# Attention steps merged into units of a head pair and half the queries, in a kernel that hides attention beside an MLP

## The chip, the core and the metric

One core of one Trainium2 chip runs the kernel. The metric is device time in microseconds (us). TensorE (PE) multiplies, ScalarE (ACT), VectorE (DVE) and GpSimd (POOL) do the elementwise work, SyncE (SP) issues all DMAs. All data are float32; the MLPs run as float32r products of high and low parts.

## The reference

Attention in two forms on q, k, v of shape (4 batches, 8 heads, 576 positions, 64), then two MLPs on 2304 x 512:

```python
q_d, k_d, v_d = (t.reshape(B, H, 144, 4, D).mean(axis=3) for t in (q, k, v))
out_d = softmax(q_d @ k_d.T / 8) @ v_d              # pooled, repeated 4 times along the positions
mask = abs(pos[:, None] - pos[None, :]) < 4
out_local = softmax(where(mask, q @ k.T / 8, -1e9)) @ v
x = (repeat(out_d, 4) + out_local) -> (2304, 512)
h = x @ w_in;  x2 = (max(h, 0) + alpha * min(h, 0)) @ w_leaky    # 512 -> 2048 -> 512
xn = x2 / rms(x2) * rms_g
y = (silu(xn @ w_gate) * (xn @ w_val)) @ w_out                   # 512 -> 1536 -> 512
```

## The kernel before

Four engines run hand-written queues that meet through semaphores. The program has these stages:

1. The first stage: attention of batch 0 by `first_order` (L1036), while SP loads w_in and w_leaky and ACT, POOL and DVE split them into a high and a low part (`piece_hi`, `piece_lo`).
2. `first_mlp` for batches 0 to 2, in a loop of three rounds (L1047). A round has 2 halves of 16 chunks. A chunk is `up` (12 matmuls, L993) and `down` (12 matmuls, L1007, two chunks behind). So a round has 64 slots, each with 12 MLP matmuls; an even slot has `up`, an odd one `down`. Ahead of a slot's MLP matmuls stand the attention steps of the next batch that `steps[s]` gives it. ACT and DVE walk the same slots: at an even slot the attention steps, then `chunk_relu` or `chunk_leaky`; at an odd one the attention steps, then `chunk_hi` or `chunk_lo`.
3. `first_mlp` for batch 3 without attention, with the weights of the second MLP coming in.
4. `second_mlp` (L1072, L1087), six blocks.

Attention has lettered steps. A (per head pair, 4 parts): transposes of q and k, copied to `qkT` by ACT (L565); DVE pools them into `qkd` (L742). B (per head, 2 parts): scores of 5 windows of 120 queries x 128 keys (L952) and of the pooled form (L955); DVE adds the mask and takes maxima (L750 to L765). P and E: exponentials on ACT (L571, L579). F: division by the sums on DVE (L770 to L777). C (per head, 2 parts): transposes of the probabilities (L961, L965), copied to `pT` and `pdT` by ACT (L586 to L591). D (per head, 2 parts): products with v (L975, L980), scaled by ACT (L597) and added into `xpair` by DVE (L789). B has 64-row operands, rows 0 to 63 for an even head and 64 to 127 for an odd one; D has 64-column results, and again a half of the partitions for each head.

Beside the MLP only PSUM banks 6 and 7 are free for attention. `in_banks` deals them out in turn, and a step that fills a bank waits until the step that filled it before has been drained (`drained`). In the first stage eight banks are dealt. The steps that fill banks (64 in a batch) are spread over slots 8 to 62 in the order of `STEPS`:

```python
        for step in order:
            steps[SLOT0 + n * (SLOT1 - SLOT0) // (len(bank_of) - 1)].append(step)
            n += 1 if USES[step[0]] and n < len(bank_of) - 1 else 0
```

Of the kernel before, what the change touches and what calls it, by code (L numbers as in the profile page):

```python
# [5 lines left out]
def attention_into_two_mlps_kernel(nc: bass.Bass, q, k, v, w_in, w_leaky, alpha, w_gate, w_val, w_out, rms_g, out):  # L6
# [23 lines left out]
    NW = 5  # L30
    QW = 120
    KSTART = [(S - P) // (NW - 1) * i for i in range(NW)]
    QSTART = [0] + [s + 4 for s in KSTART[1:-1]] + [S - QW]
    QFIRST = [0] + [KSTART[i] + QW for i in range(NW - 1)]
    QOWN = [b - a for a, b in zip(QFIRST, QFIRST[1:] + [S])]
    SPLIT = 3
    NSPLIT = sum(QOWN[:SPLIT])
    SDH = SD // 2
    PR = S // 6
# [26 lines left out]
    SPLIT_X_AFTER = ("C", 7, 1)  # L66
# [21 lines left out]
    with ctx:  # L88
# [16 lines left out]
        mask = sb("mask", [QW, NW, P], f32, part1)  # L105
# [3 lines left out]
        vwin = sb("vwin", [P, 2, NW, 2, D], f32, part1)  # L109
        v4 = sb("v4", [SDH, 4, FACTOR, D], f32, part1)  # L110
        vd = sb("vd", [SDH, 2, 4, D], f32, part1)
        sm = sb("sm", [QW, 2, NW, P], f32, part1)
        pd = sb("pd", [SDH, 2, 2, SD], f32, part1)
        pT = sb("pT", [P, NW * QW], f32, part1)
        pdT = sb("pdT", [SDH, 2, SD], f32, part1)
        negmax = sb("negmax", [QW, 4, NW], f32, part1)
        negmaxd = sb("negmaxd", [SDH, 4, 4], f32, part1)
        sums = sb("sums", [QW, 4, NW + 2], f32, part1)
        rsum = sb("rsum", [QW, NW + 2], f32, part1)
        od = sb("od", [P, SD], f32, part1)  # L120
# [5 lines left out]
        sm_first = sb("sm_first", [QW, 2, NW, P], f32, part0)  # L126
        pd_first = sb("pd_first", [SDH, 2, 2, SD], f32, part0)
        pT_first = sb("pT_first", [P, NW * QW], f32, part0)
        pdT_first = sb("pdT_first", [SDH, 2, SD], f32, part0)
# [30 lines left out]
        banks = [ctx.enter_context(nc.psum_tensor(f"bank{i}", [P, 512], f32)) for i in range(8)]  # L160
# [9 lines left out]
        s_consts = sem("s_consts")  # L170
        s_chain = sem("s_chain")
# [10 lines left out]
        s_drained = {kind: sem(f"s_drained_{kind}") for kind in "ACD"}  # L182
        s_drained_b = [sem(f"s_drained_B{j}") for j in range(2)]
        s_qkT = sem("s_qkT")
        s_qkd = sem("s_qkd")
        s_masked = sem("s_masked")
# [3 lines left out]
        s_exp = sem("s_exp")  # L190
        s_guard = sem("s_guard")
# [60 lines left out]
        USES = {"A": 4, "B": 2, "C": 2, "D": 2, "P": 0, "E": 0, "F": 0}  # L252
# [4 lines left out]
        def in_banks(order, ring):  # L257

            fills = [step for step in order if USES[step[0]]]
            return {step: (ring[n % len(ring)], fills[n - len(ring)] if n >= len(ring) else None)  # L260
                    for n, step in enumerate(fills)}
# [6 lines left out]
        for step in first_order:  # L268
            if step[0] == "F" or step[::2] == ("B", 1):
                PIECES_AFTER[step] = (n, n + 1)  # L270
                n += 2
# [6 lines left out]
        def bank(b, kind, i, j):  # L278
            return banks[(first_bank_of if isinstance(b, int) and b == 0 else bank_of)[kind, i, j][0]]


# [9 lines left out]
        def probs_of(b, i):  # L291

            buf = (i - H + 2) % depth(b, "sm")
            return (sm[:, buf], pd[:, buf], buf) if buf < 2 else (sm_first[:, buf - 2], pd_first[:, buf - 2], buf)
# [9 lines left out]
        def probsT_of(b, i):  # L304

            return ((pT, pdT), (pT_first, pdT_first))[(H - 1 - i) % depth(b, "pT")]
# [6 lines left out]
        def filled(eng, b, kind, i, j):  # L313

            eng.wait_ge(s_filled[kind], USES[kind] * ((PAIRS if kind == "A" else H) * b + i) + j + 1)

        def drained(eng, b, kind, i, j):

            if kind == "B":
                eng.wait_ge(s_drained_b[j], H * b + i + 1)  # L320
            else:
                eng.wait_ge(s_drained[kind], USES[kind] * ((PAIRS if kind == "A" else H) * b + i) + j + 1)

# [10 lines left out]
        def _(sp):  # L334
# [17 lines left out]
            def load_qk(b, p, t):  # L352

                n0, pair = H * b + 2 * p, PAIRS * b + p
                later(sp, s_filled["A"], 4 * pair - 2 + 2 * t)
                for e in range(2):
                    sp.dma_start(qk_tok[:, t, :, e, :], (qf, kf)[t][bass.ds(n0 + e, 1), :, :]
                                 .rearrange("n (p r) d -> p (n r) d", r=6)).then_inc(s_qk_in[t], 16)

            def load_v(b, p):  # L360
# [7 lines left out]
                later(sp, s_filled["D"], 4 * pair - 4)  # L368
                for i in range(NW):
                    sp.dma_start(vwin[:, p % 2, i, :, :],  # L370
                                 vf[bass.ds(n0, 2), KSTART[i]:KSTART[i] + P, :].rearrange("n p d -> p n d")
                                 ).then_inc(s_v_in[p % 2], 16)

            def store_pair(b, p):
                drained(sp, b, "D", 2 * p + 1, 1)
                sp.dma_start(x_dram[bass.ds(b * DM + p * P, P), :], xpair_of(b, p)[:, :]).then_inc(s_x_out, 16)
# [17 lines left out]
            def load_block2(i):  # L394
                if isinstance(i, int) and i == 0:
                    sp.wait_ge(s_x2_out, 16 * -(-TB2 // TB1) + BEGUN)
                    drained(sp, B - 1, "D", H - 1, 1)
# [12 lines left out]
            def after_step(b, kind, i, j, more=True):  # L410
# [3 lines left out]
                if (kind, i % 2, j) == ("D", 1, 1):  # L414
# [62 lines left out]
        def _(pool):  # L477
# [6 lines left out]
            pool.memset(sums[:, :], 1.0).then_inc(s_consts, 1)  # L484
# [4 lines left out]
            for i in range(NW):  # L489
                off = QSTART[i] - KSTART[i]  # L490
                pool.affine_select(out=mask[:, i, :], in_=mask[:, i, :], compare_op=ALU.is_gt, fill=NEG,
                                   base=FACTOR + off, pattern=[[-1, P]], channel_multiplier=1
                                   ).then_inc(s_chain, 1)
            for i in range(NW):
                off = QSTART[i] - KSTART[i]
                pool.wait_ge(s_chain, 3 + i)
                pool.affine_select(out=mask[:, i, :], in_=mask[:, i, :], compare_op=ALU.is_gt, fill=NEG,
                                   base=FACTOR - off, pattern=[[1, P]], channel_multiplier=-1
# [13 lines left out]
            def v_sums(b, p):  # L512
                pair = PAIRS * b + p
                pool.wait_ge(s_v4_in, 32 * (pair + 1) if isinstance(pair, int) else 32 * pair + 32)
                later(pool, s_filled["D"], 4 * pair - 4)
# [9 lines left out]
            for kind, i, j in first_order:  # L525
# [3 lines left out]
                if (kind, i % 2, j) == ("D", 1, 1) and i // 2 + 2 < PAIRS:  # L529
# [9 lines left out]
        def _(act):  # L539
# [5 lines left out]
            def piece_hi(n):  # L545
                wait_piece(act, n)
                i = n if n < Q1 else n - Q1
                if n >= Q1:
                    if i < Q1:
                        act.wait_ge((s_h, s_g_used)[i % 2], C1 * (NB1 - 1) + i // 2 + 1 + BEGUN)  # L550
                    elif i == Q1:
                        drained(act, B - 1, "D", H - 1, 1)
                act.activation(wpiece(i, 0), ring_slot(n)[1], ACT.Copy).then_inc(s_whi, 1)

            def attention(b, kind, i, j):
                n = H * b + i
                qkT, qkd = qk_of(b, i if kind == "A" else i // 2)
                sm, pd, buf = probs_of(b, i)
                pT, pdT = probsT_of(b, i)
                if kind == "A":  # L560

                    later(act, s_filled["B"], 4 * (PAIRS * b + i + 1 - depth(b, "qkT")))
                    filled(act, b, kind, i, j)
                    t, r0 = j // 2, 3 * (j % 2)
                    act.activation(qkT[:, t, :].rearrange("p (a r) -> p r a", r=6)[:, r0:r0 + 3, :],  # L565
                                   bank(b, kind, i, j)[:, 0:3 * PR].rearrange("p (r a) -> p r a", r=3),
                                   ACT.Copy, scale=SCALE if t == 0 else 1.0).then_inc(s_drained["A"], 1)
                if kind == "P":
                    act.wait_ge(s_dmax, n + 1)
                    for c in range(2):  # L570
                        last = act.activation(pd[:, c, :],  # L571
                                              bank(b, "B", i, 1)[0:SDH, P + SD * c:P + SD * (c + 1)],
                                              ACT.Exp, bias=negmaxd[:, buf, 2 + c:3 + c], scale=1.0 / FACTOR ** 2,
                                              accum_out=sums[0:SDH, buf, NW + c:NW + c + 1])
                    last.then_inc(s_drained_b[1], 1)
                if kind == "E":
                    act.wait_ge(s_max, n + 1)
                    for w in range(NW):
                        last = act.activation(sm[:, w, :], sm[:, w, :], ACT.Exp,  # L579
                                              bias=negmax[:, buf, w:w + 1], accum_out=sums[:, buf, w:w + 1])  # L580
                    last.then_inc(s_exp, 1)
                if kind == "C" and j == 0:

                    later(act, s_filled["D"], 2 * (n + 1 - depth(b, "pT")))
                    filled(act, b, kind, i, j)
                    act.activation(pT[:, 0:4 * QW], bank(b, kind, i, j)[:, 0:4 * QW], ACT.Copy  # L586
                                   ).then_inc(s_drained["C"], 1)
                if kind == "C" and j == 1:
                    filled(act, b, kind, i, j)
                    act.activation(pT[:, 4 * QW:5 * QW], bank(b, kind, i, j)[:, 0:QW], ACT.Copy)  # L590
                    act.activation(pdT[:, :, :], bank(b, kind, i, j)[0:SDH, QW:QW + 2 * SD], ACT.Copy  # L591
                                   ).then_inc(s_drained["C"], 1)
                if kind == "D" and j == 0:
                    e = i % 2
                    later(act, s_drained["D"], 2 * n - 2)
                    filled(act, b, kind, i, j)
                    act.activation(od[D * e:D * e + D, :], bank(b, kind, i, j)[D * e:D * e + D, NSPLIT:NSPLIT + SD],  # L597
                                   ACT.Copy, scale=1.0 / FACTOR).then_inc(s_od, 1)

            def split_x(b, half, tiles=range(KT)):  # L600
                blk = 2 * b + half
                for t in tiles:
# [4 lines left out]
                    if half == 0 and t >= KT - depth(b, "xpair"):  # L607
                        drained(act, b, "D", 2 * t + 1, 0)
# [119 lines left out]
        def _(dve):  # L728
# [6 lines left out]
            def attention(b, kind, i, j):  # L735
                n = H * b + i
# [394 lines left out]
```

## Time and profile before

| | |
|---|---|
| median of 3 runs | 1099.6 us (1097.94 to 1099.8) |
| span of the profiled execution | 1098.4 us |
| first stage | to about 81 us |
| three rounds with attention | 81.1 to 232.6, 233.1 to 382.9, 384.7 to 532.9 us |
| the MLP alone, then the second MLP | from 532.9 us |
| PE busy | 1067.3 us, 97% |
| DVE, ACT, POOL busy | 493.8, 471.9, 100.5 us |

The profiled execution lies 1.2 us below the median. PE is the bound wherever it is busy all the time; the table's ends of the rounds are read from the chain of work.

### The profile page before, as it was taken

Reading aid. Unit: us, or ns where it says so; the run is one execution under the profiler, and the core shown is the slowest. Engines: PE = TensorE matmul, PEld = TensorE weight load, DVE = VectorE, ACT = ScalarE, POOL = GpSimd, SP = SyncE. Lnnn points to the kernel's source line nnn. Section 1 sums busy time; section 2 is a strip of 40 time slices with the busy share of each in tenths; the row PEclk is TensorE's granted clock in tenths of the full one; section 3 lists DMA queues with packets and bytes.
Section 4 is the critical chain, followed back from the end, with each engine's and each line's share of the span. In section 5 each row is a group of like instructions: output and inputs, shape, how many; then the busy total and the mean of one; then the engine's idle time right before and its main releaser. Section 6 shows DMA issues by size and latency. Waiting matters only on the chain.

```text
span 1098.4 us, 19260 instructions
## 1 busy us (share of the span) xinstructions
PE 1067.3 (97%) x6837; PEld 1001.4 (91%) x6837; DVE 493.8 (45%) x916; ACT 471.9 (43%) x1335; POOL 100.5 (9%) x114
## 2 busy tenths in 40 slices
PE   6789999999999999999999999999999999999998
PEld 5679999989999899999999999999999999999997
DVE  5984555435555445554325654424224224233111
ACT  5765565545564455655435544313213222223111
POOL 5670000000000100000000122000000000000000
PEclk9969999999999999999999999999999999999999
DMA  8662122121121321210303243010100100100000
GB/s 221 188 175 67 23 78 56 51 83 41 37 55 44 85 67 23 78 35 28 93 1 99 68 136 98 9 58 1 58 0 0 57 0 0 57 0 0 29 1 30
DMA packets 105793, 61.25 MB, mean 56 GB/s; under 512 B 62036, under 2 KB 97768, under 8 KB 105704
## 3 DMA queue, kind: packets, MB, share of 16 engines
q1 hardware_dynamic: 105704, 60.11, 19.2%
q8 instruction: 50, 0.82, 0.3%
q14 instruction: 39, 0.32, 0.1%
HBM read 45.93 MB, written 14.16 MB: 55 GB/s over the span
## 4 chain that ended last, share of the span: by engine, by line
PE 94%; DVE 3%; issue 1%; ACT 1%; DMA 0%; SPq 0%; ACTq 0%; DVEq 0%
PE bank L1072 28%; PE bank L993 19%; PE bank L1007 19%; PE bank L1087 14%; PE bank L952 4%; PE bank L975 4%; PE bank L961 2%; PE bank L944 2%; PE bank L955 2%; PE bank L980 2%; PE bank L965 1%; DVE qkd L742 0%; DVE W L732 0%; ACT qkT L565 0%; DVE xlo L800 0%
## 5 line engine op out<-in xcount | busy, mean ns | idle before, releaser
L1072 PE MATMUL bank<-xnhi,W 128*128 128x384 f32 x1056 | 281.4, 339 | 0.0
L993 PE MATMUL bank<-xhi,W 128*128 128x288 f32 x1024 | 235.7, 308 | 6.4 <-issue 3.7
L1007 PE MATMUL bank<-g1hi,W 128*128 128x288 f32 x1024 | 229.9, 303 | 0.4 <-DVE g1lo L813 0.4
L1072 PEld LDWEIGHTS bank<-xnhi,W 128*128 128x128 f32 x1056 | 192.8, 188 | 2.8
L993 PEld LDWEIGHTS bank<-xhi,W 128*128 128x128 f32 x1024 | 173.9, 192 | 14.2 <-issue 10.0
L1072 PE MATMUL bank<-xnlo,W 128*128 128x384 f32 x528 | 178.4, 338 | 0.0
L1007 PEld LDWEIGHTS bank<-g1hi,W 128*128 128x128 f32 x1024 | 170.6, 188 | 6.8 <-issue 5.3
L993 PE MATMUL bank<-xlo,W 128*128 128x288 f32 x512 | 152.5, 298 | 0.0
L1007 PE MATMUL bank<-g1lo,W 128*128 128x288 f32 x512 | 151.0, 295 | 0.0
L652 ACT ACTIVATE silu<-bank 128x384 f32<-128x384 f32 x72 | 35.4, 492 | 265.0 <-PE bank L1072 265.0
L846 DVE TENSOR_TENSOR g<-bank,silu 128x384 f32<-128x384 f32 x72 | 40.1, 557 | 241.8 <-ACT silu L652 241.8
L806 DVE SCALAR_TENSOR_TENSOR pos<-neg,coef,pos 128x288 f32<-128x288 f32 x128 | 69.2, 541 | 156.3 <-ACT neg L616 155.9
L615 ACT ACTIVATE pos<-bank 128x288 f32<-128x288 f32 x128 | 52.3, 409 | 156.3 <-PE bank L993 155.5
L1087 PE MATMUL bank<-W,g2hi 128*128 128x512 f32 x360 | 113.1, 395 | 0.0
L1072 PEld LDWEIGHTS bank<-xnlo,W 128*128 128x128 f32 x528 | 99.2, 188 | 2.8
L993 PEld LDWEIGHTS bank<-xlo,W 128*128 128x128 f32 x512 | 98.9, 193 | 0.1
L1007 PEld LDWEIGHTS bank<-g1lo,W 128*128 128x128 f32 x512 | 96.6, 189 | 0.0
L622 ACT ACTIVATE g1hi<-pos 128x288 fp32r<-128x288 f32 x128 | 56.9, 444 | 56.2 <-DVE pos L806 54.7
L813 DVE TENSOR_TENSOR g1lo<-pos,g1hi 128x288 fp32r<-128x288 f32 x128 | 59.1, 462 | 47.5 <-ACT g1hi L622 46.8
L1087 PEld LDWEIGHTS bank<-W,g2hi 128*128 128x128 f32 x360 | 66.8, 188 | 10.8
L1087 PE MATMUL bank<-W,g2lo 128*128 128x512 f32 x180 | 71.1, 395 | 0.0
L849 DVE TENSOR_TENSOR g2lo<-g,g2hi 128x384 fp32r<-128x384 f32 x72 | 40.2, 558 | 42.9 <-ACT g2hi L655 42.9
(124 smaller groups left out, 1370.7 us busy)
## 6 DMA issues: line engine op xcount, KB each, us to landing
stage<-in_moe_w_out_dram SPq DMA_DIRECT2D x20, 256.0 KB, 3.0
vwin<-in_v_dram SPq DMA_DIRECT2D x80, 64.0 KB, 2.2
qk_tok<-in_q_dram SPq DMA_DIRECT2D x32, 144.0 KB, 3.0
qk_tok<-in_k_dram SPq DMA_DIRECT2D x32, 144.0 KB, 2.8
v<-in_v_dram SPq DMA_DIRECT2D x32, 144.0 KB
x_scratch<-x2sb SPq DMA_DIRECT2D x8, 576.0 KB, 3.6
xn<-x_scratch SPq DMA_DIRECT2D x6, 768.0 KB, 4.5
out_dram<-ysb SPq DMA_DIRECT2D x18, 256.0 KB, 2.0
```

The lines of the kernel that those rows point to most:

```text
L615: act.activation(pos[:, c % 2, :], hb[c % 2][:, 0:TB1], ACT.Relu).then_inc(s_pos, 1)
L622: act.activation(g1hi[:, c % 3, :], pos[:, c % 2, :], ACT.Copy).then_inc(s_ghi, 1)
L806: dve.scalar_tensor_tensor(out=pos[:, c % 2, :], in0=neg[:, c % 2, :], scalar=coef[:, c:c + 1], in1=pos[:, c % 2, :], op0=ALU.mult, op1=AL ...
L813: dve.tensor_tensor(g1lo[:, c % 3, :], pos[:, c % 2, :], g1hi[:, c % 3, :].bitcast(f32), ALU.subtract).then_inc(s_glo, 1)
L846: dve.tensor_tensor(g2[:, c % 2, :], val_b[c % 2][:, 0:TB2], silu[:, c % 2, :], ALU.mult).then_inc(s_g2, 1)
L849: dve.tensor_tensor(g2lo[:, c % 3, :], g2[:, c % 2, :], g2hi[:, c % 3, :].bitcast(f32), ALU.subtract).then_inc(s_g2lo, 1)
L952: last = pe.matmul(ab[0:QW, at:at + P], qkT[rows, 0, QSTART[w]:QSTART[w] + QW], qkT[rows, 1, KSTART[w]:KSTART[w] + P], start=True, stop=True)
L975: last = pe.matmul(ab[rows, o0:o0 + QOWN[w]], vwin[:, buf, w, e, :], pT[:, p0:p0 + QOWN[w]], start=True, stop=True)
L993: last = pe.matmul(hb[c % 2][:, 0:TB1], w, x[:, t, :], start=(t + j == 0), stop=(t == KT - 1 and j == 2))
L1007: last = pe.matmul(acc[t][:, 0:TB1], w, g[:, c % 3, :], start=(c == 0 and j == 0), stop=(c == C1 - 1 and j == 2))
L1072: last = pe.matmul(bank[:, 0:TB2], w, x[:, t, :], start=(t + j == 0), stop=(t == KT - 1 and j == 2))
L1087: last = pe.matmul(y_b[t][:, :], g, wpiece(piece, w), start=(c == 0 and j == 0), stop=(c == C2 - 1 and j == 2))
```

## The change

- The unit of B, P, E, F, C and D is now a head pair and half of the queries (288), still 8 units in a batch (`U`), two for a pair. A half has 3 windows (`WH`) of 96 queries x 102 keys, and 72 pooled queries.
- B, C and D have one part instead of two (`USES`). B and C are wide: they take a pair of banks, one for each head, starting at an even bank (`WIDE`, `in_banks`, `bank_pair`). Beside the MLP a wide step takes both free banks, so it waits for every step before it, and the next step waits for it.
- In a burst of B or D all matmuls of the even head come first, then those of the odd one (in D: windows of head 0, windows of head 1, pooled products of head 0, of head 1).
- DVE: one mask addition of 2 x 450 elements out of both banks, one pooled maximum out of SBUF (288), one local maximum (612); in F one tensor for both heads; in D one addition of 288 elements on 128 partitions in place of two, of 344 and 232, on 64. ACT: 6 exponentials of 102 elements for E in place of 5 of 128; P reads and writes SBUF; one copy of 2 x 432 elements in C in place of three; D scales 72 elements on 128 partitions. P and E now both write `sm`.
- q and k are loaded so that A's copies are contiguous (`(r p)` for `(p r)`); 6 windows of v are loaded for a pair in place of 5. `split_x` of half 0 waits for the unit 2t only.

40 steps now fill banks, over the same slots 8 to 62. Worked out from the code, some slots are:

| slot | before | after |
|---|---|---|
| 24 to 27 | C1.1 / B3.0 / B3.1 P3 D1.0 / D1.1 | P2 F1 D0 / none / E2 F2 C1 / B3 |
| 28 to 31 | E3 F3 C2.0 / C2.1 / A2.0 / A2.1 | P3 D1 / none / E3 F3 C2 / A2.0 |
| 48 to 50 | B6.1 / P6 D4.0 / D4.1 E6 F6 C5.0 | D3 / E5 C4 / F5 B6 |
| 57 to 60 | E7 F7 D6.0 / D6.1 / C7.0 / C7.1 | C6 / none / E7 F7 D6 / C7 |

The core of the diff:

```diff
-    NW = 5
-    QW = 120
+    HALF = S // 2
+    QW = 96
+    WH = HALF // QW
+    NW = 2 * WH
+    KW = QW + 2 * (FACTOR - 1)
...
-        USES = {"A": 4, "B": 2, "C": 2, "D": 2, "P": 0, "E": 0, "F": 0}
+        USES = {"A": 4, "B": 1, "C": 1, "D": 1, "P": 0, "E": 0, "F": 0}
+        WIDE = "BC"
...
+            before, at, last_in = {}, 0, {}
+            for step in order:
+                if not USES[step[0]]:
+                    continue
+                wide = step[0] in WIDE
+                at += at % 2 if wide else 0
+                taken = [ring[(at + k) % len(ring)] for k in range(1 + wide)]
+                before[step] = taken, list(dict.fromkeys(last_in[k] for k in taken if k in last_in))
+                last_in.update((k, step) for k in taken)
+                at += 1 + wide
+            return before
...
@@ scalar @@
+                    for e in range(2):
+                        for w in range(WH):
+                            own = sm[:, e, w * KW:(w + 1) * KW]
+                            last = act.activation(own, own, ACT.Exp, bias=negmax[:, buf, e, w:w + 1],
+                                                  accum_out=sums[:, buf, e, w:w + 1])
...
+                if kind == "C":
+                    later(act, s_filled["D"], n + 1 - depth(b, "pT"))
+                    filled(act, b, kind, i)
+                    act.activation(probsT_of(b, i)[:, :, :], bank_pair(b, kind, i)[0:KW, :, 0:TW], ACT.Copy
...
@@ vector @@
+                    dve.tensor_tensor(sm[:, :, 0:SCORES], bank_pair(b, kind, i)[0:QW, :, 0:SCORES],
+                                      mask[:, i % 2, :].unsqueeze(1).to_broadcast([QW, 2, SCORES]), ALU.add
+                                      ).then_inc(s_drained["B"], 1)
+                    drained(dve, b, kind, i)
+                    dve.tensor_reduce(negmaxd[:, buf, 0, :], sm[:, :, LOCAL:SCORES], axis=AX.X, op=ALU.max,
+                                      negate=True).then_inc(s_dmax0, 1)
+                    dve.tensor_reduce(negmax[:, buf, :, :], local, axis=AX.X, op=ALU.max, negate=True
+                                      ).then_inc(s_max, 1)
...
@@ tensor @@
+                for step in before:
+                    drained(pe, b, *step)
...
+                    for e in range(2):
+                        for w in range(WH):
+                            q0, k0 = h * HALF + w * QW, KSTART[h * WH + w]
+                            pe.matmul(scores[0:QW, e, w * KW:(w + 1) * KW], qkT[rows[e], 0, q0:q0 + QW],
+                                      qkT[rows[e], 1, k0:k0 + KW], start=True, stop=True)
+                        qd = qkd[rows[e], :, :].rearrange("p t s -> p (t s)")[:, h * SDH:h * SDH + QW]
+                        last = pe.matmul(scores[0:QW, e, LOCAL:SCORES], qd, qkd[rows[e], 1, :], start=True, stop=True)
...
+                    for e in range(2):
+                        for w in range(WH):
+                            pe.matmul(ab[D * e:D * e + D, w * QW:(w + 1) * QW], vwin[:, vbuf, h * WH + w, e, :],
+                                      pT[:, e, w * QW:(w + 1) * QW], start=True, stop=True)
+                    pe.wait_ge(s_vd, PAIRS * b + i // 2 + 1)
+                    for e in range(2):
+                        for kc in range(2):
+                            last = pe.matmul(ab[D * e:D * e + D, TQ:TQ + SDH], vd[:, vbuf, 2 * kc + e, :],
+                                             pT[0:SDH, e, TQ + kc * SDH:TQ + (kc + 1) * SDH],
+                                             start=(kc == 0), stop=(kc == 1))
```

## Rows read from the trace of the kernel before

**Rows 1.** Busy us (x instructions), clock, DMA of two stretches: first stage, third round.
```profile
core 0: us, PE busy (x) PEld busy (x) DVE busy (x) ACT busy (x) POOL busy (x), PEclk, DMA share, GB/s
20.00:76.00 56.00, 44.55 (x277) 39.84 (x274) 53.96 (x92) 44.24 (x164) 40.10 (x36) 0.85 0.69 193
384.67:532.90 148.23, 147.65 (x1114) 138.50 (x1115) 75.97 (x166) 80.64 (x266) 4.84 (x6) 1.00 0.16 45
```

**Rows 2.** Chain of work (start us, us, what): round boundary, and undisturbed MLP.
```profile
230.97 2.16 issue
233.13 6.56 PE bank L993 x36
...
532.90 4.77 PE bank L993 x36
```

**Rows 3.** The same chain: both parts of one head's B.
```profile
256.52 1.06 PE bank L952 x8
257.58 1.78 PE bank L1007 x12
259.37 0.41 PE bank L952 x2
259.77 0.49 PE bank L955 x4
```

**Rows 4.** The same chain: both parts of one head's D.
```profile
220.82 0.73 PE bank L975 x6
221.55 0.49 PE bank L980 x4
...
223.84 0.54 PE bank L975 x4
```

**Rows 5.** The same chain: one head's C, and the MLP matmuls behind it.
```profile
267.88 0.41 PE bank L961 x4
...
270.00 0.25 PE bank L965 x4
270.25 1.65 PE bank L1007 x12
```

**Rows 6.** Timeline of PE (start us, us, what): neighbouring heads side by side.
```profile
17.79 1.91 PE L952 MATMUL bank<-qkT 64*120 64x128 f32 x8
19.49 0.44 PE L955 MATMUL bank<-qkd 64*72 64x144 f32 x1
19.50 0.56 PE L952 MATMUL bank<-qkT 64*120 64x128 f32 x1
...
74.98 0.26 PE L975 MATMUL bank<-pT_first,vwin 128*64 128x112 f32 x1
74.98 0.32 PE L975 MATMUL bank<-pT,vwin 128*64 128x120 f32 x1
...
75.62 0.66 PE L980 MATMUL bank<-pdT,vd 72*64 72x144 f32 x4
```

**Rows 7.** Timeline of PE: the first B of a round, with the idle time before it.
```profile
250.92 1.13 PE L952 MATMUL bank<-qkT 64*120 64x128 f32 x8 [0.59 <-DVE qkd L742]
```

**Rows 8.** Timeline of ACT: the first and the last of an E's five windows.
```profile
258.21 0.39 ACT L579 ACTIVATE sm<-sm,negmax 120x128 f32<-120x128 f32 x1
...
260.04 0.19 ACT L579 ACTIVATION_READ_ACCUMULATOR sm<-sm,negmax 120x1 f32 x1
```

**Rows 9.** Timeline of DVE: the first instruction of an F, and the one behind it.
```profile
261.72 0.16 DVE L770 TENSOR_SCALAR sums<-sums 120x7 f32<-120x7 f32 x1
...
263.26 0.51 DVE L806 SCALAR_TENSOR_TENSOR pos<-neg,coef,pos 128x288 f32<-128x288 f32 x1
```

**Rows 10.** Groups by line and shape (count, busy us, mean ns, idle before).
```profile
L615 ACT ACTIVATE pos<-bank 128x288 f32<-128x288 f32 x128 | 52.3, 409 | 156.3 <-PE bank L993 155.5 <-DVE g1lo L813 0.6
L586 ACT ACTIVATE pT<-bank 128x480 f32<-128x480 f32 x28 | 15.8, 564 | 8.7 <-PE bank L961 8.7
L765 DVE TENSOR_REDUCE negmax<-sm 120x5 f32<-120x640 f32 x28 | 23.0, 820 | 0.0
L750 DVE TENSOR_TENSOR sm<-bank,mask 120x512 f32<-120x512 f32 x28 | 19.3, 688 | 8.7 <-PE bank L952 8.5
```

More of the change, by code:

```diff
@@ L158, in attention_into_two_mlps_kernel @@
         part2.close()
-        banks = [ctx.enter_context(nc.psum_tensor(f"bank{i}", [P, 512], f32)) for i in range(8)]
+        two_banks = [ctx.enter_context(nc.psum_tensor(f"banks{i}", [P, 2, 512], f32)) for i in range(4)]
+        banks = [two_banks[i // 2][:, i % 2, :] for i in range(8)]
         acc = banks[0:4]
@@ L488, in _ @@
             pool.wait_ge(s_chain, 2)
[L489 to L492, printed above, removed]
+            for w in range(NW):
+                off, own = QW * w - KSTART[w], mask[:, w // WH, w % WH * KW:(w % WH + 1) * KW]
+                pool.affine_select(out=own, in_=own, compare_op=ALU.is_gt, fill=NEG,
+                                   base=FACTOR + off, pattern=[[-1, KW]], channel_multiplier=1
                                    ).then_inc(s_chain, 1)
[L494 to L498, printed above, removed]
+            for w in range(NW):
+                off, own = QW * w - KSTART[w], mask[:, w // WH, w % WH * KW:(w % WH + 1) * KW]
+                pool.wait_ge(s_chain, 3 + w)
+                pool.affine_select(out=own, in_=own, compare_op=ALU.is_gt, fill=NEG,
+                                   base=FACTOR - off, pattern=[[1, KW]], channel_multiplier=-1
                                    ).then_inc(s_consts, 1)
@@ L569, in attention @@
                     act.wait_ge(s_dmax, n + 1)
[L570 to L575, printed above, removed]
+                    for e in range(2):
+                        last = act.activation(sm[:, e, LOCAL:SCORES], sm[:, e, LOCAL:SCORES], ACT.Exp,
+                                              bias=negmaxd[:, buf, 1, e:e + 1], scale=1.0 / FACTOR ** 2,
+                                              accum_out=sums[:, buf, e, WH:WH + 1])
@@ L587, in attention @@
                                    ).then_inc(s_drained["C"], 1)
[L588 to L598, printed above, removed]
+                if kind == "D":
+                    later(act, s_drained["D"], n)
+                    filled(act, b, kind, i)
+                    act.activation(od[:, :], bank(b, kind, i)[:, TQ:TQ + SDH], ACT.Copy, scale=1.0 / FACTOR
+                                   ).then_inc(s_od, 1)
@@ L967, in attention @@
                 if kind == "D":
-                    e, buf = i % 2, i // 2 % 2
-                    rows = slice(D * e, D * e + D)
-                    drained(pe, b, "C", i, 1)
-                    pe.wait_ge(s_v_in[buf], 16 * NW * (PAIRS // 2) * b + 16 * NW * (i // 4 + 1))
-                    for w in (range(0, SPLIT), range(SPLIT, NW))[j]:
-                        o0 = QFIRST[w] - (NSPLIT if j else 0)
-                        p0 = w * QW + QFIRST[w] - QSTART[w]
-                        last = pe.matmul(ab[rows, o0:o0 + QOWN[w]], vwin[:, buf, w, e, :],
-                                         pT[:, p0:p0 + QOWN[w]], start=True, stop=True)
@@ L977, in attention @@
-                    if j == 0:
-                        pe.wait_ge(s_vd, PAIRS * b + i // 2 + 1)
+                    vbuf, ab = i // 2 % 2, bank(b, kind, i)
+                    drained(pe, b, "C", i)
+                    pe.wait_ge(s_v_in[vbuf], 16 * NW * (PAIRS // 2) * b + 16 * NW * (i // 4 + 1))
+                    for e in range(2):
+                        for w in range(WH):
+                            pe.matmul(ab[D * e:D * e + D, w * QW:(w + 1) * QW], vwin[:, vbuf, h * WH + w, e, :],
+                                      pT[:, e, w * QW:(w + 1) * QW], start=True, stop=True)
@@ L979, in attention @@
+                    pe.wait_ge(s_vd, PAIRS * b + i // 2 + 1)
+                    for e in range(2):
                         for kc in range(2):
[L980 to L981 removed]
+                            last = pe.matmul(ab[D * e:D * e + D, TQ:TQ + SDH], vd[:, vbuf, 2 * kc + e, :],
+                                             pT[0:SDH, e, TQ + kc * SDH:TQ + (kc + 1) * SDH],
+                                             start=(kc == 0), stop=(kc == 1))
@@ L1036, in _ @@
             for step in first_order:
-                if first_bank_of.get(step) == (3, None):
+                taken, before = first_bank_of.get(step, ([], []))
+                if 3 in taken and not before:
                     pe.wait_ge(s_coef, 3)
```

231 lines of the change are left out of this document (96 added, 135 removed).

## The prediction, made before the changed kernel was run

> **What bounds the kernel now.** I first read the busy times by stretch [rows 1]. In the third round PE is busy 147.65 of 148.23 us, DVE and ACT about half of it: a round is as long as PE's queue. In the first stage it is DVE that is busy, 53.96 of 56 us. The change touches these two stages; from 532.9 us on nothing changes. Then I read the chain of work, which in a round is PE's queue with a price on each burst. 36 MLP matmuls take 4.77 us, so a slot's 12 take 1.59 [rows 2], and the 64 slots 101.8 of the 148.2 us. Attention and what it does to its neighbours is the rest, 46.4 us a round.
>
> **PE's bursts before.** B's first part is 8 records in 1.06 us, the second 2 records in 0.41 and 4 pooled ones in 0.49 [rows 3]. 8 records in 1.06 and 2 in 0.41 give 0.108 us a record and 0.19 us at the start of a burst. The MLP matmuls behind a B take 1.78 us instead of 1.59, another 0.19: entering and leaving the 64-row shape costs 0.38 us. A head's B in two slots costs 1.06 + 0.41 + 0.49 + 2 x 0.19 = 2.34 us. D is 0.73 + 0.49 in the first part and 0.54 in the second [rows 4]; I take 0.19 behind each as for B: 2.14 us. For the start of a D, 6 records with 344 columns in 0.73 and 4 with 232 in 0.54 give some 0.15 us, and 0.084 us for 100 columns. C is 0.41 + 0.10 + 0.25, and 0.06 behind it [rows 5], 0.82 us. 8 heads of B and D make 8 x (2.34 + 2.14) = 35.8 us; three times in a round two bursts stand together (both parts of B2, both of D3, the second of B3 with the first of D1), which saves about 0.3 each: 34.9.
>
> **PE's bursts after.** A record's time goes with its columns. B: 102 columns are 0.108 x 102/128 = 0.086 us; a head has 6 of these and 2 pooled ones of 0.49/4 = 0.12, 0.76 us. D: 96 columns are 0.081 us and 72 are 0.061; a head has 6 and 4, 0.73 us. C: 6 transposes of 0.41/4 x 96/120 and 4 of 0.06 are 0.74, with 0.06 behind it 0.80.
>
> The question is whether the two heads of a burst run one after the other or side by side. The trace has both shapes [rows 6]. At 19.49 us the last four records of one head's B run (the pooled ones) and at 19.50 the next head's begin, on the other 64 rows; each keeps its own pace. But they did not begin earlier, beside the 8 records from 17.79 on, though their operands were there. At 74.98 us the last four records of one head's D and the first six of the next begin together, and at 75.62 all ten are through: 0.64 us, the time of six. So heads run side by side, and in both places the second begins when four records of the first are left. I take this as the look ahead. Then B is 4 records alone (0.34) and the other head's 0.76: 1.10 us; with 0.38 for the shape, 1.48. D is 2 records alone (0.16) and 0.73: 0.89; with 0.15 + 0.19, 1.23. 8 of each are 21.7 us a round. Full overlap would be 1.14 and 1.07; none, 1.90 and 1.80.
>
> Saved on PE: 34.9 - 21.7 + 0.2 for C = 13.4 us a round, 40.2 in three. A's transposes keep their columns and count. Of the 13.4, some 14 bursts fewer are about 5; overlap is nearly all of the rest.
>
> The Trainium skill, "TensorE: Matmul & The Clock Gate", Part 3, says that a weight load overlaps with running matmuls only when the row group differs. D's two heads differ in columns, not rows, so by it D would not gain, 1.80 and not 1.23. The row at 74.98 us speaks against it; it is the third rival below.
>
> **What the wide steps add: waits for a bank.** Before, a step waited for the step before the last one; PE's idle in the third round is 0.58 us, all but nothing of it on banks (0.59 is the wait of a round's first B for the pooled q and k [rows 7], which I leave in place though its copy gets shorter). After, B and C need both banks, and the next step needs them drained. I walk the slots at which ACT has an E ahead of C's copy. E now: 5 windows run in 260.23 - 258.21 = 2.0 us less a last overlap of 0.1, 0.385 each [rows 8]; 102 elements instead of 128 give about 0.365, six 2.2 us. C's copy: 288 elements 409 ns, 480 elements 564, so 0.81 ns an element, and 864 elements 0.88 us [rows 10]. F lasts 1.54 us [rows 9] and hardly changes. Times below are from the end of the slot's last `up`.
> - Slots 26 and 27, before B3: relu, leaky and hi (0.41 and 0.3 for the relus, 0.5, 0.4 with their hand-overs) free ACT at 1.7; E2 to 3.9; C1's copy to 4.8. PE has a down 1.6, C1 0.74, an up 1.65: it stands at 4.0. Wait 0.85. Slots 30 and 31, before A2: the same, 0.85.
> - Slots 49 and 50, before B6: ACT relu to 0.75, E5 to 2.95, C4's copy to 3.85. PE: C4 and a down, 2.4. Wait 1.45.
> - Slots 59 and 60, before C7: E7 to 2.95, F7 on DVE to 4.5, D6's addition to 4.95. PE: D6 and a down, 2.85. Wait 2.1.
> - Elsewhere a slot's 1.6 to 1.8 us covers the drain: B's mask addition has 900 elements at (820 - 688)/128 = 1.03 ns above 688 ns for 512, 1.09 us [rows 10]; D's drain is 0.3 + 0.45. A fill never shares a slot with another now.
>
> Sum 5.3 us a round, 15.9 in three. Behind the waiting PE stand only MLP matmuls whose inputs ACT and DVE made two chunks ahead, so these engines catch up meanwhile. Bounds: 0, if ACT runs ahead further than my walk lets it, and 1.6 us at each of the 16 wide steps, 25.6 a round, if their drains run into the next slot throughout.
>
> **The clock.** At the round boundary at 231 us PE was idle for 2.16 us and 36 matmuls behind it took 6.56 us instead of 4.77, so 1.8 us were lost to the lower of the two levels [rows 2]; the other waits of the walk are shorter. I put 1.5 us for C7's three waits, between 0 and 1.8 for each of twelve.
>
> **The first stage.** DVE sets it [rows 1]. Per unit its additions for D lose 288 elements and an instruction, 0.30 + 0.16; mask addition, 640 elements in two to 900 in one, gains 0.27 - 0.16; the maxima and F lose 28 elements each, 0.06. Net 0.41, times 8 is 3.3 us; I take 3, between 0 (if the DMAs, busy 0.69, come last instead) and 5 (with D's shorter tail ahead of the first `up`). The six v loads for five and the two memsets of POOL hide beside 0.31 of free DMA time and before the first mask. SP's queue has fewer steps to pass. ACT's A copies become contiguous, which I leave out.
>
> **Sum.** 1098.4 - 40.2 + 15.9 + 1.5 - 3 = 1072.6 us; the profiled execution is 1.2 below the median, so 1073.8.
>
> **The rivals.**
> 1. Full overlap: the look ahead is no limit when the queue stands ready. 0.34 and 0.16 less per unit are 4 us a round, 12 in three: 1062. For it: a semaphore may have held back the head at 74.98. Against it: none did at 17.79.
> 2. No overlap, so that the blocks do not do what they are laid out for: (1.90 - 1.48) + (1.80 - 1.23) = 0.99 per unit, 7.9 a round, less 0.6 that C7's wait gives back: +22, 1096. For it: within one program step heads never stood side by side before, and D's two now write one bank.
> 3. D alone does not overlap: 0.57 x 8 - 0.57 = 4.0 a round: 1086.
> 4. The clock falls at all twelve long waits: 12 x 1.8 - 1.5 = +20: 1094.
> 5. Slower: the drains become the chain. One mechanism: ACT and DVE carry a backlog from unit to unit, and each of the 16 wide steps in a round waits for one slot, 1.6 us. That is 25.6 for 5.3 a round: +61, 1135. It decides from (13.4 + 1)/16 = 0.9 us per wide step. Against it: ACT and DVE are busy 81 and 76 of 148 us [rows 1].
>
> **How the numbers follow.** Chances: forecast 0.42, rival 1 0.14, 2 0.13, 3 0.10, 4 0.09, 5 0.09; 0.03 for losses that just cancel the gain. The range runs from 1059 (rival 1 with shorter waits) to 1096 (rival 2), leaving out rival 5, the 0.03 and some 0.08 of tails. Faster by over 0.2% (2.2 us, about what a measurement of this kernel can tell from no change): 0.88; within: 0.03; slower: 0.09.
>
> **What would show it.** In the chain of the changed kernel: B bursts near 1.3 us with the start and D near 1.04, with records of both heads starting together; starts with no overlap at all would mean rival 2 or 3. Idle PE ahead of B3, A2.0, B6 and C7 of 0.85, 0.85, 1.45, 2.1, released by ACT's `pT` and DVE's `xpair` or `sm`; more places would mean rival 5. A round near 148.2 - 13.4 + 5.3 = 140 us; the first stage 3 us shorter; MLP slots at 1.59 except behind B and D. The prediction is wrong if records in small shapes have a floor above 0.06 to 0.09 us, which no row reaches with 64-column results.

## The result, and the profile after

The changed kernel takes 1086.5 us (median of 4 runs, 1083.57 to 1086.65) for 1099.7: ratio 0.9875, 95% interval 0.9855 to 0.9896. 1073.8 was predicted: a gain of 25.9 us was forecast and 13.2 was measured. The profiled execution has a span of 1081.7 us and took 1083.57 in all, 2.9 us less than the median; the span of a second profile (`changed_again`, below) is 1086.3.

Where the rounds begin and end, in the chain of work of the changed kernel (start us, us, what; the rows that answer to [rows 2]):

```profile
78.56 5.69 PE banks L1000 x36
...
223.66 5.05 PE banks L1000 x36
...
371.28 5.06 PE banks L1000 x36
...
515.96 4.80 PE banks L1000 x36
```

I cut each profiled execution at the end of its first block of `up` (here 84.25 us) and at the end of the third round (515.96). All kernels of this study, in us; each row but the last column is one execution:

| kernel | first stage | three rounds | rest | span | median |
|---|---|---|---|---|---|
| before | 87.7 | 445.2 | 565.5 | 1098.4 | 1099.7 |
| changed | 84.3 | 431.7 | 565.7 | 1081.7 | 1086.5 |
| changed_again | 88.4 | 432.3 | 565.7 | 1086.3 | 1085.0 |
| c_before_e | 87.0 | 442.4 | 565.6 | 1095.1 | 1096.9 |
| e7_earlier | 86.1 | 426.6 | 565.6 | 1078.3 | 1079.5 |
| both_orders | 86.5 | 435.3 | 565.7 | 1087.4 | 1088.9 |
| turns | 87.0 | 416.5 | 565.8 | 1069.3 | 1072.2 |
| replanned | 88.2 | 415.2 | 565.7 | 1069.1 | 1070.4 |
| replanned_turns | 86.1 | 401.7 | 565.7 | 1053.5 | 1055.7 |
| f3_later | 85.7 | 397.6 | 565.7 | 1049.0 | 1051.6 |
| b_same_rows | 90.8 | 443.5 | 565.7 | 1099.9 | 1099.7 |
| before_merged | 87.1 | 454.3 | 565.5 | 1106.9 | 1109.0 |
| before_contiguous | 87.5 | 443.2 | 565.5 | 1096.2 | 1097.7 |

The change gained 13.5 us in the rounds, where 22.8 were predicted. PE's waits in the first round of the changed kernel (engine, line, releaser: total us, times, longest):

```profile
PE banks L968 <- DVE xpair L794: 2.6, 2, 2.3
PE banks L958 <- ACT pT L605: 2.2, 2, 1.4
PE banks L948 <- ACT pT L605: 0.9, 1, 0.9
PE banks L958 <- DVE qkd L755: 0.3, 1, 0.3
```

They are the waits of the walk: C7 2.3 (2.1 forecast), B6 1.4 (1.45), B3 0.8 and A2 0.9 (0.85 each), and the first B 0.3 in place of [rows 7]. A fifth wait, 0.28 us ahead of C6, was not forecast. The third round has the same four lines, beside the idle time at its own start.

The bursts, from the chain of the same round; the answer to [rows 3] and [rows 4]:

```profile
101.58 0.78 PE banks L958 x8
102.52 0.19 PE banks L958 x3
102.71 0.24 PE banks L961 x2
102.96 1.80 PE banks L1000 x12
...
122.60 0.70 PE banks L981 x10
123.46 0.25 PE banks L986 x5
123.71 1.80 PE banks L1000 x12
```

B takes 102.96 - 101.58 = 1.38 us with its start, D 1.11, and the MLP behind either 1.80. Inside a B (timeline of PE in two windows of 0.06 and 0.07 us, at 246.87 and 246.93, each with the records that are running in it; L958 are windows, L961 pooled):

```profile
246.64 0.42 PE L958 MATMUL banks<-qkT 64*96 64x102 f32 x4
...
246.65 0.41 PE L958 MATMUL banks<-qkT 64*96 64x102 f32 x3
246.81 0.28 PE L961 MATMUL banks<-qkd 64*96 64x144 f32 x1
246.90 0.25 PE L958 MATMUL banks<-qkT 64*96 64x102 f32 x1
246.94 0.28 PE L961 MATMUL banks<-qkd 64*96 64x144 f32 x1
```

The burst begins at 246.21, and one head's window records start 0.09 us apart after the first. Two start 0.01 us apart, at 246.64 and 246.65: the fifth record of the even head and the first of the odd one. The pooled records at 246.81 and 246.94 are the even head's last; windows run on between them, and these are the odd head's. So the second head runs beside the last four records of the first and not earlier, as [rows 6] had it.

### The profile page after: what moved, and what is told of

Same layout as the page of the kernel before. It is cut to its first block, busy times and chain, and to the rows that moved or that the text cites. A ratio compares the mean times of both kernels' runs of the same rounds, so it can differ in the third digit from the quotient of the medians.

```text
span 1081.7 us, 19528 instructions
## 1 busy us (share of the span) xinstructions
PE 1034.1 (96%) x7125; PEld 979.7 (91%) x7125; DVE 484.0 (45%) x852; ACT 457.5 (42%) x1335; POOL 99.7 (9%) x117
## 4 chain that ended last, share of the span: by engine, by line
PE 87%; ACT 5%; DVE 5%; issue 2%; DMA 0%; SPq 0%; ACTq 0%; DVEq 0%
PE banks L1080 28%; PE banks L1000 18%; PE banks L1014 17%; PE banks L1095 14%; PE banks L958 3%; ACT sm L598 2%; PE banks L981 2%; PE banks L948 1%; PE banks L968 1%; PE banks L961 1%; PE banks L986 1%; ACT pT L605 1%; DVE qkd L755 1%; PE banks L972 0%; DVE W L745 0%
## 5 line engine op out<-in xcount | busy, mean ns | idle before, releaser
L1080 PE MATMUL banks<-xnhi,W 128*128 128x384 f32 x1056 | 281.4, 339 | 0.0
L1000 PE MATMUL banks<-xhi,W 128*128 128x288 f32 x1024 | 233.9, 305 | 3.3 <-issue 3.3
L1014 PE MATMUL banks<-g1hi,W 128*128 128x288 f32 x1024 | 228.4, 301 | 0.4 <-DVE g1lo L817 0.4
L1080 PEld LDWEIGHTS banks<-xnhi,W 128*128 128x128 f32 x1056 | 192.8, 188 | 2.8
L1000 PEld LDWEIGHTS banks<-xhi,W 128*128 128x128 f32 x1024 | 174.0, 191 | 7.0 <-issue 5.3
L1080 PE MATMUL banks<-xnlo,W 128*128 128x384 f32 x528 | 178.4, 338 | 0.0
L1014 PEld LDWEIGHTS banks<-g1hi,W 128*128 128x128 f32 x1024 | 171.1, 189 | 4.3 <-issue 3.8
L1000 PE MATMUL banks<-xlo,W 128*128 128x288 f32 x512 | 152.9, 299 | 0.0
L1014 PE MATMUL banks<-g1lo,W 128*128 128x288 f32 x512 | 151.7, 296 | 0.0
L1095 PE MATMUL banks<-W,g2hi 128*128 128x512 f32 x360 | 113.1, 395 | 0.0
```

Source lines behind the costliest of these rows:

```text
L1000: last = pe.matmul(hb[c % 2][:, 0:TB1], w, x[:, t, :], start=(t + j == 0), stop=(t == KT - 1 and j == 2))
L1014: last = pe.matmul(acc[t][:, 0:TB1], w, g[:, c % 3, :], start=(c == 0 and j == 0), stop=(c == C1 - 1 and j == 2))
L1080: last = pe.matmul(bank[:, 0:TB2], w, x[:, t, :], start=(t + j == 0), stop=(t == KT - 1 and j == 2))
L1095: last = pe.matmul(y_b[t][:, :], g, wpiece(piece, w), start=(c == 0 and j == 0), stop=(c == C2 - 1 and j == 2))
```

## The experiments

### turns: does a second head have to wait for the first?

The first of these hunks stands in B and again in D, the second in D alone; in B the pooled matmuls then follow all windows, one for each head.

```diff
-                    for e in range(2):
-                        for w in range(WH):
+                    for w in range(WH):
+                        for e in range(2):
...
-                    for e in range(2):
-                        for kc in range(2):
+                    for kc in range(2):
+                        for e in range(2):
```

> The changed kernel with the matmuls of a burst of B or D in turns: window 0 of head 0, window 0 of head 1, window 1 of head 0 and so on. Theory (the second head begins only when four records of the first are left): the second head now begins after two records at most, so B's burst of 1.38 us becomes about 1.05 and D's of 1.11 about 0.95, 0.33 + 0.16 for 24 units: span 1081.7 - 12 = 1070 us, within 3. Rival (turns cost something on each change of head, or the look ahead is no limit): bursts as long as before or longer, span 1081 to 1090.

Ratio to before 0.9764 (0.9741 to 0.9787), span 1069.3. The chain:

```profile
244.39 0.70 PE banks L958 x12
245.09 0.25 PE banks L962 x4
245.34 1.79 PE banks L1001 x12
...
264.55 0.65 PE banks L982 x12
265.20 0.25 PE banks L987 x8
265.45 1.81 PE banks L1001 x12
```

B is 0.95 us instead of 1.38, D 0.90 instead of 1.11: 0.64 for 24 units is 15.4 us, and the three rounds are 15.2 us shorter. The agreement is closer than it should be: PE's waits for banks grew by 2.9 us (C7's from 2.3 to 2.5, C6's from 0.3 to 0.9), and the clock fell once in place of three times. The bursts themselves are somewhat shorter than expected, and they are the full overlap of rival 1: two heads in the time of one. The limit was the order in which they were issued.

### b_same_rows: is it the rows that let them overlap?

```diff
-                    scores, rows = bank_pair(b, kind, i), [slice(D * e, D * e + D) for e in range(2)]
+                    scores, rows = bank_pair(b, kind, i), [slice(0, D) for e in range(2)]
```

> The changed kernel with the odd head's B read from rows 0 to 63 too, so that both heads of a burst stand on the same rows of the array (the odd head's scores are then those of the even one, which is wrong, and as much work). Theory (heads run side by side because they stand on different rows): B's burst is 0.19 + 16 records one after another, 1.80 us for 1.38: 24 x 0.42 = 10, span 1092 us, within 3. Rival (the burst is short for its fewer records alone): 1081 to 1084.

Ratio 0.9982 (0.9962 to 1.0001), span 1099.9. The chain has the heads one behind the other:

```profile
258.56 0.69 PE banks L958 x6
259.26 0.24 PE banks L961 x2
259.50 0.53 PE banks L958 x6
260.03 0.25 PE banks L961 x2
260.28 1.79 PE banks L1000 x12
```

B is 1.72 us, 0.34 more; the rounds are 11.8 us longer. The span of 1092 that was expected was missed by 8 us. 24 x 0.34 = 8.2 of it is the bursts, and the clock fell six times instead of twice or three times (slots of 2.7 to 2.8 us behind the waits for B6 and C7), which makes the rest. The first stage came out at 90.8 us, the longest of all; its share of 6.5 over the changed kernel's profile, or 2.4 over its second, I cannot put down to B alone. The rival fell: B's overlap in blocks is worth 8 us of the change's gain of 13 in the rounds. No run takes D's overlap away. As an estimate, 20 records of 0.081 and 0.061 us one after another and a start of 0.17 would make D 1.63 us for 1.11, another 12 us in 24 units.

### before_merged: what does merging give without overlap?

```diff
-            steps[SLOT0 + n * (SLOT1 - SLOT0) // (len(bank_of) - 1)].append(step)
-            n += 1 if USES[step[0]] and n < len(bank_of) - 1 else 0
+            steps[SLOT0 + n * (SLOT1 - SLOT0) // 39].append(step)
+            n += 1 if USES[step[0]] and (step[0] == "A" or step[2] == 1) and n < 39 else 0
```

> The kernel before with nothing but both parts of a B, C or D put into one slot: 40 places over slots 8 to 62, as in the changed kernel, heads one by one. PE enters and leaves the small shapes 13 times less in a round, 13 x 0.36 = 4.7 us, 14 in three. C's copies still stand behind an E on ACT, so the waits ahead of B3, A2.0, B6 should come here too, somewhat shorter because two banks are drained one by one: 2 to 3 us a round; and C7 behind D6, 2. Forecast span 1098.4 - 14 + 12 = 1096 us, within 4. If merging itself made the gain of the change, 1085 or less.

Ratio 1.0069 (1.0052 to 1.0086), span 1106.9: 0.7% slower than before, and 11 us over the forecast. PE's waits in its first round, without that for `xlo`, which belongs to the first stage:

```profile
PE bank L961 <- DVE xpair L789: 1.7, 1, 1.7
PE bank L961 <- ACT pd L571: 1.1, 1, 1.1
PE bank L952 <- ACT pT L586: 1.0, 2, 0.8
PE bank L944 <- ACT pd L571: 1.0, 1, 1.0
PE bank L952 <- DVE qkd L742: 0.6, 1, 0.6
PE bank L944 <- ACT pT L586: 0.3, 1, 0.3
```

The waits ahead of B3, A2, B6 (L952, L944 for `pT`) and C7 are here as foreseen. Two more I had not seen: C3 and A1 wait for P (`pd`), which in this kernel still reads the bank of B. In the changed kernel P reads `sm`, and these two waits of 1.1 and 1.0 us are absent; that is a part of the change which the prediction gave no worth. By the waits the rounds lose 14.6 us more than before's. Three falls of the clock (slots of 2.7 to 2.9 us, each with one of 2.0 to 2.2 behind it) cost 1.5 us each. Together this ate more than the 14 us that merging was to save. All three falls stand behind B6's wait of 0.8 us, and none behind C7's of 1.7.

### c_before_e, e7_earlier, both_orders: taking the waits away, first try

From here to f3_later a diff shows only the stretches of the string `STEPS` that differ. PE's own order of work stays as it is; ACT and DVE walk theirs otherwise.

```diff
-D0 E2 F2 C1 B3 P3 D1 E3 F3 C2 A2
+D0 C1 E2 F2 B3 P3 D1 C2 E3 F3 A2
...
-D3 E5 C4 F5 B6
+D3 C4 E5 F5 B6
```

> The changed kernel with C ahead of E in the order of the steps at three places (C1 before E2, C2 before E3, C4 before E5); PE's own order is the same, only ACT and DVE walk it otherwise. Theory (the waits ahead of B3, A2 and B6 come from C's copy standing behind an E on ACT): the waits of 0.8, 0.9 and 1.4 us a round go, 9.4 us in three rounds, and with the wait ahead of B6 the fall of the clock behind it in one round (1.5 us). Profiled span 1081.7 - 11 = 1071 us, within 3. Rival (ACT is full in these slots, so the wait only moves): PE idles as long as before at other steps, span 1080 to 1084.

Ratio 0.9964 (0.9948 to 0.998), span 1095.1: 13 us longer than the changed kernel's first profile, 9 than its second, where 11 less were expected. PE's longest waits in its three rounds:

```profile
PE banks L968 <- DVE xpair L794: 9.3, 6, 2.3
PE banks L981 <- DVE sm L763: 8.8, 6, 2.5
PE banks L1014 <- DVE g1lo L817: 4.7, 3, 1.6
...
```

The waits for C's copy (`pT`) are gone, and D now waits for B's mask addition (L763) and a `down` for `g1lo`. The chain of one of these places:

```profile
282.84 2.02 ACT sm L598 x11
284.95 0.18 DVE sums L777
...
286.10 0.45 DVE sm L785
286.55 1.02 DVE sm L763
287.61 0.77 PE banks L981 x10
...
288.92 3.17 PE banks L1000 x12
```

E2 starts later because ACT first waits for C1; F2 waits for E2, and on DVE B3's addition stands behind F2. I had looked only at the queue in which the wait arose and not at the next one. The clock fell six times, as in the last line (3.17 us for 12 matmuls).

```diff
-B7 P7 D5 C6 E7 F7 D6 C7 D7
+B7 P7 D5 E7 C6 F7 D6 C7 D7
```

> The changed kernel with E7 ahead of C6 in the order of the steps, two slots earlier. Theory (the wait ahead of C7 is the chain E7, F7, D6's addition): the wait of 2.3 us a round goes, 6.9 us, and the two falls of the clock right behind it, 1.4 us each. Profiled span 1081.7 - 9.7 = 1072 us, within 3. Rival (the wait moves to D6 or C7 behind C6's copy, now behind E7): span 1079 to 1084.

Ratio 0.9815 (0.9798 to 0.9831), span 1078.3, rounds 5.1 us shorter: half of what was expected. C7's wait shrank from 2.3 to 1.2, 1.8 and 0.5 in the three rounds, for F7 had stayed behind in slot 59.

> Both moves together. Theory: no wait of PE for a bank over 0.5 us is left in a round, the clock stays at its upper level between the round boundaries: span 1081.7 - 16.3 - 4.3 = 1061 us, within 4. If the clock falls without the long waits too, 1065; if the waits move, over 1072.

Ratio 0.9908 (0.9882 to 0.9934), span 1087.4. The fault of the first edit stayed (8.8 us for L763), so 1061 was missed by 26.

### replanned and replanned_turns: the walk through both queues

```diff
-D0 E2 F2 C1 B3 P3 D1 E3 F3 C2 A2
+D0 C1 E2 B3 F2 P3 D1 C2 E3 F3 A2
...
-D3 E5 C4 F5 B6 P6 D4
+D3 C4 E5 B6 F5 P6 D4
...
-B7 P7 D5 C6 E7 F7 D6 C7 D7
+B7 P7 D5 E7 F7 C6 D6 C7 D7
```

> The changed kernel with its step order so planned that neither engine's queue holds a bank's drain behind an E or an F: C1 ahead of E2, but F2 behind B3 (the first try with C ahead of E had F2 ahead of B3, and D1 waited 2.5 us for B3's addition behind it on DVE), C2 ahead of E3, C4 ahead of E5 with F5 behind B6, and E7 and F7 two slots earlier. PE's order of work is the same. Theory (all idle PE inside a round is a drain queued behind an E or an F): no wait for a bank over 0.5 us in a round, 16 us of 18 gone, and the clock stays up, 4: span 1081.7 - 20 = 1061 us, within 5. Rival (ACT and DVE are short of time between slots 23 and 60, so the waits only move, as in the first try): over 1072.

Ratio 0.9721 (0.9695 to 0.9748), span 1069.1. PE's waits in the second round:

```profile
PE banks L1014 <- DVE g1lo L817: 1.6, 1, 1.6
PE banks L958 <- DVE qkd L755: 0.3, 1, 0.3
```

All bank waits are gone from the round, with PE's queue unchanged, and no slot shows the lower clock; one wait of 0.8 us ahead of C7 is left in the first round. The wait for `g1lo` is new: the changed kernel has none, c_before_e has it too. The rounds are 16.5 us shorter, and most of it adds up: 16.1 us of bank waits and some 4.3 of clock less, 4.7 of the new wait more. 20 were expected. The rest of the miss (1069 for 1061) is the first stage, 88.2 us here. So the bank waits and the falls behind them, which the sum had at 17.4 us, are nearly all removable by order alone, at the price of the new wait.

> The same order of steps and the matmuls of a burst in turns. Theory: both savings add, since one shortens PE's own work and the other its waits: 1061 - 11 = 1050 us, within 5. Rival (shorter bursts leave ACT and DVE less time and waits come back): 1055 to 1065.

Ratio 0.9577 (0.9556 to 0.9598), span 1053.5: the rounds lose 16.5 us by the order, another 13.5 by the turns. Alone, the turns gave 15.2, so both nearly add: 30.0 for 31.7.

### f3_later: the wait for `g1lo`

```diff
-D1 C2 E3 F3 A2 D2 B4 P4 C3
+D1 C2 E3 A2 D2 F3 B4 P4 C3
```

> The replanned order with turns, and F3 behind D2 instead of ahead of A2. In the replanned order PE waits 1.6 us once a round for a low part of the first MLP (a down), because on DVE F3, which waits for E3, stands ahead of it. Theory: that wait goes, 4.7 us in three rounds: span 1053.5 - 4.7 = 1049 us, within 3; the three rounds, from the end of the first block of up to the end of the third round, take 397 us for 401.7. Rival (C3 then waits for F3 behind B4's addition): 1052 to 1056.

Ratio 0.9572 (0.9532 to 0.9611), median 1051.6, span 1049.0; rounds 397.6. The wait for `g1lo` fell from 4.7 to 1.8 us in three rounds:

```profile
PE banks L1015 <- DVE g1lo L817: 1.8, 3, 0.6
...
```

This is the fastest kernel of the study, 35 us under the changed one. Beside replanned_turns its gain of 4 us in both span and rounds is about the size of the intervals, and only 2.9 of it are the wait. Another 1.5 are the clock: behind one round boundary replanned_turns has 36 matmuls in 6.57 us, where this kernel has 5.06. That 1049 was met is in part luck.

### changed_again: the first stage

> The changed kernel itself once more, for its first stage. In the profile of it the first block of up ended at 84.3 us, in four kernels with the same first stage at 86.1 to 88.2, in the kernel before at 87.7. Theory (the first stage varies by some 3 us from run to run, and the change saves no more than 1 us there): 86 to 88 us here, and a span of 1084 to 1086. Rival (84.3 is the kernel's own, and the others differ by their orders or chip): 84 to 85, span 1082.

Ratio 0.9862 (0.9822 to 0.9903), span 1086.3, and in the chain

```profile
81.75 6.61 PE banks L1000 x27
```

the first block ends at 88.4 us. The rounds agree with the first profile (432.3 and 431.7). So 84.3 was a short first stage. The six executions with the changed kernel's first stage lie from 84.3 to 88.4, 86.7 in the mean, where before has 87.7.

### before_contiguous: one part alone

```diff
-                                 .rearrange("n (p r) d -> p (n r) d", r=6)).then_inc(s_qk_in[t], 16)
+                                 .rearrange("n (r p) d -> p (n r) d", r=6)).then_inc(s_qk_in[t], 16)
...
-                    act.activation(qkT[:, t, :].rearrange("p (a r) -> p r a", r=6)[:, r0:r0 + 3, :],
-                                   bank(b, kind, i, j)[:, 0:3 * PR].rearrange("p (r a) -> p r a", r=3),
+                    act.activation(qkT[:, t, r0 * PR:(r0 + 3) * PR], bank(b, kind, i, j)[:, 0:3 * PR],
```

> The kernel before with one part of the change: q and k loaded by (r p), so that A's copies on ACT are contiguous. A copy takes 0.41 us for 0.73. Theory: only the wait of a round's first B gets shorter, 0.59 to 0.28, and the start of the first stage, where two copies stand in the chain, 0.6: span 1098.4 - 1.5 = 1097 us, within 2. Rival (ACT's 0.32 us less on 16 copies, or the other DMA pattern, moves the first stage by more): outside 1095 to 1099.

Ratio 0.9988 (0.9966 to 1.001), span 1096.2, PE's wait for the first `qkd` 0.8 us in three rounds: as expected, and within what can be told from no change.

## Why the prediction was right, and where its terms were off

The direction and the range held (1059 to 1096), the time was 12.7 us too low, and the gain half of what was forecast. 9.1 of the 12.7 us are in the span, the other 3.6 in how the profiled execution stands to the median, which the sum had at 1.2 us. By its steps:

- **PE's bursts, look ahead of four records: right in kind, 0.20 us a unit too short.** B is 1.38 and not 1.29, D 1.11 and not 1.04, and the MLP behind them 1.80, not 1.78. The first record of each head takes 0.16 us and not 0.09 before the next one starts. From the third round, 144.7 - 101.9 - 6.0 of waits - 1.8 of clock leaves 35.0 us of attention, where the sum had 45.8 - 13.4 = 32.4. 1.6 of the 2.6 are the bursts. The rest is in small pieces of 0.2 us: C7's transposes, which took 0.97 us in place of 0.76; the three bursts of B behind a wait (0.85 instead of 0.78 for the first eight records); A2's first transposes behind theirs (0.46 instead of 0.25); the round's first `down` (1.85 us, before 1.64); and the other C's, 0.02 each. In three rounds 7.8 us, the largest term of the miss.
- **The waits: right.** 6.0 us a round measured, 5.3 and 0.59 forecast, at the four places named, released by the lines named. replanned shows the cause, since PE's queue did not change in it. One duration in the walk was right by luck: the slope for B's mask addition came from two different instructions, a reduction of 640 elements (L765) and an addition of 512 (L750), and gave the 1.09 us that the addition then took.
- **The clock: too small.** 1.5 us were set for it; the profile of the changed kernel shows three falls. In the chain of its second round:

```profile
356.08 0.43 PE banks L968 x3
356.51 0.13 PE banks L972 x2
356.64 0.41 PE banks L968 x3
357.05 0.24 PE banks L972 x2
357.29 2.91 PE banks L1000 x12
360.20 1.61 PE banks L1014 x12
```

  Behind C7's wait of 2.4 us C itself slows down (0.41 and 0.24 for the second head, at full pace 0.25 and 0.13) and 12 matmuls take 2.91 us instead of 1.64. With one more behind C7 in the third round and one behind B6's wait of 1.4 us (2.83 and 2.07) it is 4.3 us, 2.8 more than set. Rival 4 had them at all twelve waits; they came at three in this execution and at two in changed_again, where one of them cost 2.9 us.
- **The round boundary:** behind one of its boundaries before ran 36 matmuls in 6.56 us, at a granted clock of 0.66 from 233.1 to 236 us; behind the other it took 5.03, as the changed kernel did behind both (5.05 and 5.06, at 1.00). The sum did not have this 1.5 us. It comes and goes with the execution, so it is no effect of the change: before_contiguous has 5.03 at both boundaries, and replanned_turns and both_orders have 6.57 and 6.56 at one.
- **The first stage: 3 us set, 3.4 in one execution and -0.7 in the other.** DVE is busy 49.6 of the 56 us from 20 to 76 where it was 53.96 [rows 1], so its work did shrink as worked out; but it is then no longer the whole chain. In the chain of changed_again PE's bursts stand in it for most of the time from 37 to 75 us, and at half pace (three transposes of 96 columns in 0.65 us, which take 0.25 in a round). Over the six executions the stage is 0.9 us shorter than in the one of before. The bound of 0 was the better guess.
- **Sum for the rounds:** 22.8 - 7.8 - 2.8 + 1.5 = 13.7; measured 13.5 and 12.9. The forecast missed by no more than this because the boundary's 1.5 us went the other way.

Rival 1 (full overlap) fell for blocks and holds for turns; rival 2 (none) fell with b_same_rows. Rival 3 fell as well: D's heads differ in columns alone, and D takes 0.90 us in turns with its start, where its 20 records one after another would take 1.46 without it. Rival 3 rested on the rule of the Trainium skill, "TensorE: Matmul & The Clock Gate", Part 3, that a weight load overlaps with running matmuls only when the row group differs; the measurement decides against it here. Rival 5 did not come about, though c_before_e shows how near it lay: three steps moved in two queues brought the change's gain in the rounds down by four fifths, from 13.5 to 2.8 us.

What stays open: why the second head starts just when four records are left, what decides behind which waits the clock falls, and what makes the first stage vary by 4 us.

## What to carry to other kernels

Merging steps shortens PE's own work by sharing the cost of entering and leaving a small shape, but on two banks each step that takes both waits for every drain before it; walk the drain through every engine's queue, the one behind it too, before the steps are ordered. Small matmuls on different rows or columns of the array should be issued in turns and not in blocks: here that alone nearly doubled the gain. When an order is changed to take a wait away, compare PE's waits by releaser in both traces; a wait that goes and one that comes look alike in the span.

## What the runs showed of the hardware

- Two heads on different 64-row or 64-column parts run at full pace side by side: B 0.95 us for 0.76 of one head's records and 0.19 of start, D 0.90 for 0.73 and 0.17 (turns). With both heads on the same rows B takes 1.72 us (b_same_rows).
- In blocks the second head starts when four records of the first are left: seen record by record in B (246.65 us), and in D by the length of its burst (1.11 us; the walk with four records gave 1.04).
- PE idle for 0.8 to 2.5 us is sometimes followed by a fall of the granted clock to the lower of its two levels (0.57 from 503 to 507 us in the changed kernel), at a cost of some 1.5 us, once 2.9. The length of the wait doesn't decide it: in before_merged the clock fell in all three rounds behind 0.83 us and never behind 1.65. All 26 falls inside the rounds of these thirteen executions followed a wait with a B, C or D right behind it; the twelve waits of 1.6 us ahead of a `down` had none (c_before_e, both_orders, replanned, replanned_turns).
- In the first stage the granted clock of the profile and the pace of PE don't agree. From 20 to 76 us it reads 1.00 in the changed kernel and 0.54 in turns, yet both ran three transposes at the same pace there, 0.65 us for the 0.25 of a round:

```profile
20.00:76.00 56.00, 40.55 (x299) 36.33 (x300) 49.59 (x78) 42.26 (x160) 38.43 (x37) 1.00 0.77 201
54.79 0.65 PE banks L968 x3
...
20.00:76.00 56.00, 35.41 (x302) 30.66 (x304) 49.79 (x76) 40.82 (x153) 37.95 (x35) 0.54 0.76 198
55.43 0.65 PE banks L969 x3
```

  The first two lines are of the changed kernel, the others of turns: the busy times of [rows 1] and a line of the chain. So a clock of 1.00 in that stage is no proof of full pace; compare the time of a shape that also stands in a round.
